# First batch's attention in four rounds of query tiles, with token chunks of 128, 128, 128 and 192 behind them

## The reference, cut to what matters

```python
# attention: batch 4, 8 heads, sequence 576, head size 64, float32
scores = q @ k.T / sqrt(64)
cum = cumsum(max(s, 0))
scores = where(causal, -1e9, scores + min(-(cum_q - cum_k), 0))
attn = softmax(scores)
x = attn @ v                                     # 2304 tokens x 512
# first dense stage, 512 -> 768 -> 512
h = max(x @ w1, x @ w2, x @ w3);  y = h @ w_out
# second dense stage, 512 -> 1536 -> 512
out = ((y @ w_a) * (y @ w_b)) @ w_out2
```

## Time and profile before

| | |
|---|---|
| median of 3 runs | 985.52 us (985.21 to 985.62) |
| the profiled execution's own time | 985.47 us |
| its span (first to last instruction) | 983.7 us |
| PE busy | 941.9 us, 96% of the span |
| DVE, ACT, POOL busy | 468.9, 406.6, 202.9 us |
| matmuls | 5776 |

### The profile page before, as it was taken

One profiled execution on the slowest core, in us unless ns is written; L12 is line 12 of the kernel. 1 busy time (PEld: TensorE's weight loads), 2 busy tenths in 40 slices (PEclk: granted clock), 3 DMA queues, 4 the chain that ended last, 5 costly groups with the idle time before them and its releaser, 6 DMA issues.

```text
span 983.7 us, 15197 instructions
## 1 busy us (share of the span) xinstructions
PE 941.9 (96%) x5776; PEld 858.7 (87%) x5776; DVE 468.9 (48%) x1054; ACT 406.6 (41%) x912; POOL 202.9 (21%) x293
## 2 busy tenths in 40 slices
PE   3688999999999999999999999999999999999998
PEld 2578899999999999999999888888888888888898
DVE  6689978877666577563323433221122112211222
ACT  4677777766655566543223333211121112111211
POOL 5556554444423324411000000000000000000000
PEclk9999999999999999999999999999999999999999
DMA  3544432222121221100032332100020001000100
GB/s 103 149 158 153 147 97 64 71 77 78 57 86 39 80 69 40 54 9 27 12 134 69 120 97 91 66 21 1 0 72 14 1 1 64 1 1 1 43 1 22
DMA packets 29240, 58.74 MB, mean 60 GB/s; under 512 B 3184, under 2 KB 15568, under 8 KB 29136
## 3 DMA queue, kind: packets, MB, share of 16 engines
q1 hardware_dynamic: 29168, 57.77, 18.6%
HBM read 47.87 MB, written 9.88 MB: 59 GB/s over the span
## 4 chain that ended last, share of the span: by engine, by line
PE 88%; DVE 5%; issue 4%; DMA 1%; POOL 1%; ACT 0%; SPq 0%; POOLq 0%; ACTq 0%; DVEq 0%
PE bank L1129 30%; PE bank L1008 21%; PE bank L1144 15%; PE bank L1027 8%; PE bank L960 5%; PE bank L990 5%; PE bank L976 4%; DVE soft L754 1%; DVE pt_lo L763 1%; DVE h_lo L794 1%; DVE qk_st L726 1%; DVE w_lo L732 1%; DMA cum_dram<-cum_row 0%; DVE qk_st L720 0%; DMA qk_raw<-in_qk 0%
## 5 line engine op out<-in xcount | busy, mean ns | idle before, releaser
L919 DVE TENSOR_TENSOR g_raw<-bank,a_sb 128x512 f32<-128x512 f32 (+1 forms) x60 | 38.3, 639 | 298.5 <-PE bank L1129 298.5
L1008 PE MATMUL bank<-xs_hi,w_hi 128*128 128x256 f32 (+1 forms) x576 | 173.9, 302 | 2.2 <-DVE xs_lo L775 1.5
L1008 PE MATMUL bank<-xs_hi,w_lo 128*128 128x256 f32 (+1 forms) x576 | 170.7, 296 | 0.0
L1008 PE MATMUL bank<-xs_lo,w_hi 128*128 128x256 f32 (+1 forms) x576 | 170.6, 296 | 0.0
L458 POOL TENSOR_SCALAR soft<-soft,rden 128x576 f32<-128x576 f32 (+4 forms) x160 | 102.7, 659 | 236.6 <-DVE rden L740 236.6
L1129 PE MATMUL bank<-y_hi,w2b_hi 128*128 128x512 f32 (+1 forms) x360 | 132.4, 368 | 0.0
L1129 PE MATMUL bank<-y_lo,w2b_hi 128*128 128x512 f32 (+1 forms) x360 | 132.4, 368 | 0.0
L1129 PE MATMUL bank<-y_hi,w2b_lo 128*128 128x512 f32 (+1 forms) x360 | 132.4, 368 | 0.0
L500 ACT ACTIVATE soft<-soft,neg_max 64x576 f32<-64x576 f32 (+4 forms) x160 | 96.1, 601 | 45.8 <-DVE neg_max L754 45.0
L1008 PEld LDWEIGHTS bank<-xs_hi,w_hi 128*128 128x128 f32 x576 | 109.3, 190 | 3.7 <-DVE xs_lo L775 1.7
L665 ACT ACTIVATE a_sb<-bank 128x512 f32<-128x512 f32 (+1 forms) x60 | 33.3, 555 | 188.5 <-PE bank L1129 188.5
(11 more groups left out here) (83 smaller groups left out, 1821.9 us busy)
## 6 DMA issues: line engine op xcount, KB each, us to landing
qk_raw<-in_qk SPq DMA_DIRECT2D x32, 576.0 KB, 3.8
w_raw<-in_w SPq DMA_DIRECT2D x40, 384.0 KB, 3.5
v_raw<-in_v SPq DMA_DIRECT2D x32, 160.0 KB, 2.2
y_raw<-y_dram SPq DMA_DIRECT2D x4, 1024.0 KB, 5.5
outT<-o_stage SPq DMA_DIRECT2D x16, 256.0 KB, 2.0
qk_raw<-in_qk SPq DMA_DIRECT2D x8, 256.0 KB, 3.1
y_dram<-m_tmp SPq DMA_DIRECT2D x8, 160.0 KB, 1.8
y_dram<-h_raw SPq DMA_DIRECT2D x8, 160.0 KB, 1.8
```

The costliest lines, as they stand in the source:

```text
L1008: ins = nc.tensor.matmul(up_ps[g][:, 0:width1(c)], up1_w(w, f, g, kc), x[:, kc, 0:width1(c)], start=(kc == 0 and at == 0), stop=(kc == KC ...
```

## The change

- The first batch's heads run in four rounds: jobs 0 to 7 take tile 0, 8 to 15 tile 1, 16 to 23 tile 2, 24 to 31 tiles 3 and 4. The full heads are jobs 32 to 55. There are 65 slots.
- The first batch's tokens become four chunks of 128, 128, 128 and 192. They start at slots 9, 17, 25 and 33, 8 slots each (`DENSE` is 4). So the fourth chunk stands beside the full heads of batch 1. The chunks of the other batches are as before, from slot 41 on, and again beside the same heads.
- q, k and v loads, copies and splits take only the keys that the round needs. A head of the first batch is loaded four times instead of twice.
- w1 has no ring: `w1_raw` has room for all pieces, in the place where `w1_lo` lies, so the low part is written over the raw one. The high copy stays on ACT; DVE subtracts 512 of 768 columns, POOL the other 256, ahead of its normalising. The pieces are spread over slots 1 to 12.
- SP loads the bias of the first 8 jobs from SBUF and no longer waits for the store of the cumulative sums at the start.
- Jobs with one tile alternate between the two score banks. In slots without dense work ACT makes the k/q copy first, and DVE splits q and k ahead of the pt subtractions.

```diff
-EARLY_TILES, LATE_TILES = (0, 1), (2, 3, 4)
+STAGES = [(0,), (1,), (2,), (3, 4)]
+PARTIAL = HEADS * len(STAGES)
+N_JOBS = PARTIAL + N_HEADS - HEADS
...
-CHUNK = [((0, SPLIT), (SPLIT, SEQ))[c % 2] for c in range(N_CH1)]
+CHUNK = [(0, P), (P, SPLIT), (SPLIT, 3 * P), (3 * P, SEQ)] + [(0, SPLIT), (SPLIT, SEQ)] * (BATCH - 1)
...
-FIRST = [9, 17, 25, 29, 33, 37, 41, 45]
+FIRST = [9, 17, 25, 33, 41, 45, 49, 53, 57, 61]
...
-DENSE = 2
+DENSE = len(STAGES)
...
-W1_PIECES = {2: [0], 4: [1], 8: [2, 3], 9: [4, 5], 10: [6, 7], 11: [8, 9], 12: [10, 11], 13: [12, 13], 14: [14, 15]}
+W1_PIECES = {n: [n - 1] for n in range(1, 8)}
+W1_PIECES.update({8: [7, 8], 9: [9, 10], 10: [11, 12], 11: [13, 14], 12: [15]})
...
+            with ExitStack() as early:
+
+                w1_raw = early.enter_context(nc.sbuf_tensor("w1_raw", [P, W1_COLS], F32))
             w1_lo = sb("w1_lo", [P, W1_COLS], F32R)
...
-            w1_raw = [sb(f"w1_raw{r}", [P, PIECE], F32) for r in range(2)]
...
-        def score_at(i):
+        def score_at(n, i):
+            if len(tiles(n)) == 1:
+                return BANK * (n % 2)
             return PARTED if i == QT - 1 else BANK * (i % 2)
...
             sp.dma_start(cum_dram, cum_row[:, :, :].bitcast(F32)).then_inc(cum_stored, 16)
-            sp.wait_ge(cum_stored, 16)
...
+            def w1_rest_sub(piece):
+                pool.wait_ge(w1_hi_done, piece + 1)
+                cols = slice(piece * PIECE + W1_SHARE, (piece + 1) * PIECE)
+                nc.gpsimd.tensor_tensor(w1_lo[:, cols], w1_raw[:, cols], w1_hi[:, cols].bitcast(F32), ALU.subtract
+                                        ).then_inc(w1_rest_done, 1)
...
                     split_v(n)
+                for piece in W1_PIECES.get(n, []):
+                    w1_rest_sub(piece)
                 if live(n):
                     for k in range(len(tiles(n))):
                         normalise(n, k)
...
             def w1_lo_sub(piece):
                 dve.wait_ge(w1_hi_done, piece + 1)
-                cols = slice(piece * PIECE, (piece + 1) * PIECE)
+                cols = slice(piece * PIECE, piece * PIECE + W1_SHARE)
...
-                if i == QT - 1 or k == 0:
+                if i == QT - 1 or k == 0 and len(tiles(n)) > 1:
                     need(pe, neg_done, TB[n] + k)
...
-                for lo, hi in ((0, SPLIT), (SPLIT, SEQ)):
-                    if lo >= last or hi <= first:
+                for lo, hi in ((first, min(last, SPLIT)), (max(first, SPLIT), last)):
+                    if lo >= hi:
                         continue
```

More of the change, by code:

```diff
@@ L62, in live, with keys @@
     return 0 <= n < N_JOBS
-N_CH1 = 2 * BATCH
-CHUNK = [((0, SPLIT), (SPLIT, SEQ))[c % 2] for c in range(N_CH1)]
+def keys(n):
+    return KEYS[tiles(n)[-1]]
+CHUNK = [(0, P), (P, SPLIT), (SPLIT, 3 * P), (3 * P, SEQ)] + [(0, SPLIT), (SPLIT, SEQ)] * (BATCH - 1)
+N_CH1 = len(CHUNK)
 WIDE = SEQ - SPLIT
@@ L73, with batch @@
 STEPS = 6
-FIRST = [9, 17, 25, 29, 33, 37, 41, 45]
+FIRST = [9, 17, 25, 33, 41, 45, 49, 53, 57, 61]
 N_SLOTS = FIRST[-1] + 4
-DENSE = 2
+DENSE = len(STAGES)
+def batch(c):
+    return max(0, (c - 2) // 2)
 def place(n):
@@ L107, in rest_of @@
     c, e = place(n)
-    return c if c is not None and e == 0 and c in (0, 1, 2, 4, 6) else None
+    return c if c is not None and e == 0 and (c < DENSE or c % 2 == 0) else None
 def ahead_of(n):
@@ L724, in split_k @@
                 dve.wait_ge(lower_done, x + 1)
-                hi = KEYS[tiles(x)[-1]]
+                hi = keys(x)
                 nc.vector.tensor_tensor(qk_st[x % 2][DH:P, 3, 0:hi], qk_raw[x % 2][DH:P, 0:hi],
@@ L1049, in ups @@
                     up_part(c, f, g)
-            scores(0, 0)
-            scores(0, 1)
+            for k in first_scores(0):
+                scores(0, k)
             def alone_slot(n):
@@ L1057, in alone_slot @@
                     transposes(m, k)
-                if tile_count(n) > 2:
-                    scores(n, 2)
                 if live(m):
                     output(m)
-                scores(n + 1, 0)
-                scores(n + 1, 1)
+                for k in first_scores(n + 1):
+                    scores(n + 1, k)
             def share(n, at):
@@ L1101, in slot @@
                     output(m)
-                if live(n + 1):
-                    scores(n + 1, 0)
-                    scores(n + 1, 1)
+                for k in first_scores(n + 1):
+                    scores(n + 1, k)
             for n in range(N_SLOTS):
```

113 lines of the change are left out of this document (58 added, 55 removed).

## The result

The changed kernel takes **1164.09 us** (median, 1163.26 to 1164.99), the kernel before 985.57 (985.21 to 985.63) on the same chip: a ratio of 1.1812 [1.1792, 1.1833], 178.5 us slower. The forecast was 1050, with a range that ended at 1068. The direction was right. The loss was 2.8 times the 64.3 us of the sum.

A forecast was written before the change was run, and what follows sets the result against it. PE was taken to bound the kernel, short of work only before 222 us. Slots 0 to 40 summed to 285.6 us against 221.3, so 985.5 + 64.3 gave 1050 us, range 1028 to 1068.

The forecast's parts named there:

- the sum: Slot lengths added up to the end of slot 40: 285.6 us against 221.3 now, +64.3, with everything behind unchanged.
- The sign: Whole kernel slower: +57 us of PE work against 63 us idle; slower by over 0.2% given 0.97.
- a matmul under some 230 columns costs 0.11 us, whatever its width: Dense matmuls of narrow chunks: the weight load's step sets 0.11 us each; up and down matmuls of batch 0 +50.4 us.
- The 0.8 for the dropped wait: Start, first slot: SP's dropped wait, less one more weight piece ahead of the loads, brings first output 0.8 earlier, at 15.6.
- the ring of 3.7: Slots 1 to 7: w1 copy, DVE and POOL subtractions in turn, normalise, transpose, copy and handovers take 3.7 us a slot.
- rival 3: Dearer handovers, and no early start from unringed w1 because POOL's share precedes normalising: about 21 us more, 1071; chance 0.17.
- the forecast's other ring: Slots 1 to 7: SP issues five loads a slot, each v load held until v is split; some 3.4 us.
- The wait behind w1: Slots 9 to 12: next transposes wait for normalising behind two w1 pieces, 2.75 us in a slot of 5.9.
- Both waits of the forecast: Slots 25 to 32: PE waits 1.1 us for DVE's mask of tile 3 and 0.8 before the output; slot 8.8.
- about 1 in eight slots: Slots with tiles 3 and 4: PE's mask waits at L960 would be about 1 us in each of eight slots.
- rival 2: Slots 17 to 40: ACT and DVE keep pace, only PE counts; 28 us less, 1022, half 1036; chance 0.16 with half.
- The clause on 81 ns: Narrow matmuls: at the skill's 81 ns, a slot's 36 would take 2.9 us, a little under a microsecond less.

The follow-up runs named there:

- wide256: Changed kernel with the dense matmuls of the first batch's four chunks run over 256 columns, the extra ones unread; 1061.45 us, ratio 1.0768.
- nowait: Kernel before, with SP's wait for the store of the cumulative sums dropped and the first 8 jobs' bias from SBUF; 985.96 us, ratio 1.0002.
- wide256_dve: wide256 with the w1 subtraction wholly on DVE and none on POOL; 1061.12 us.
- warm: Changed kernel with 24 matmuls of 512 columns, result unread, put at the start of slot 9; 1085.76 us, one run.
- wide192: Changed kernel with the dense matmuls of its 128-token chunks run over 192 columns; 1058.98 us, ratio 1.0754.
- three192: three with its middle chunk of 128 tokens run over 192 columns; 1029.16 us, ratio 1.0440.
- three: Changed kernel with three rounds (tiles 0 and 1; 2; 3 and 4) and first-batch chunks of 256, 128 and 192 tokens; 1063.76 us, ratio 1.0797.

## Why the prediction was right and wrong

**The sign** rested on one count: PE gets 57 us more work and has 63 us idle, so even without any idle time the gain is 6 us. That held in every kernel with more chunks: 1029, 1059, 1061, 1064 and 1086, all slower.

**The step that failed** is the sentence "a matmul under some 230 columns costs 0.11 us, whatever its width", and ahead of it "2.4 GHz, the granted clock of these stretches". The clock was read from stretches of 256- and 320-column matmuls and taken along to chunks of 128 columns as if it were a property of the chip. In the runs it went with the matmuls: of 864 with 128 columns nearly all took 0.213 in the changed kernel, at half the clock; padded to 256 columns, all but the first 33 ran at the high clock, save for 3.4 us. No rival had it: each varied widths, chains and handovers, at one clock. So the range had no room for it.

The table sets the forecast beside `wide256`, which has the high clock almost throughout, and the kernel after (us; outputs by time, the rest by length).

| | forecast | wide256 | after |
|---|---|---|---|
| first output | 15.6 | 16.66 | 16.47 |
| eighth output | 41.8 | 42.47 | 42.08 |
| slot 9 | 8.4 | 9.8 | 9.9 |
| slots 10 to 12, each | 5.9 | 5.7 | 9.3 |
| slots 13 to 16, each | 4.9 | 5.2 | 9.35 |
| slots 17 to 24 | 43.9 | 47.3 | 83.1 |
| slots 25 to 32 | 70.4 | 75.0 | 115.2 |
| slots 33 to 40 | 83.8 | 86.35 | 85.4 |
| end of slot 40 | 285.6 | 298.9 | 401.0 |

**Where the missing 115 us are** (401.0 less 285.6). In slots 9 to 32 there are 24 x 36 = 864 dense matmuls, at 0.213 instead of 0.11: 89 us. The rest of these slots, attention and waits, takes 89.5 us (273.5 less 864 x 0.213), where the forecast had 65.0 (160.0 less 864 x 0.11): 24.5 more. How that splits is an estimate, since busy time is modelled. The forecast's 65.0 were 43 of PE's attention work (0.9, 1.3 and 3.1 a slot) and 22 of waits. By its busy time PE was idle for 7 us of these slots. So the attention work took some 82 us, nearly twice the 43, as at half the clock, and 15 us of the waits vanished behind the slower PE. Slots 33 to 40, at the high clock, and the start add 2. That makes 115. The split between attention's own operations isn't measured.

**What the slots said point by point.**

- *First output* 16.47 for 15.6. The 0.8 for the dropped wait does not exist: `nowait` stays at 16.38. And the change's order puts the third head's load, behind the w1 piece and the store, ahead of the first output (ScalarE waits 4.28 us for it, until 14.90), which the forecast put at nothing. It read the DMA share as under 0.5 in the earlier trace rows; the row of the start has 0.52.
- *Slots alone*: 3.2 to 4.2 for the ring of 3.7, eighth output 0.3 from the forecast. So rival 3's claim that unringed w1 brings no early start is refuted. But the ring itself isn't confirmed: without POOL's share (`wide256_dve`) it should have been 3.2, and the eighth output came at 42.5 as with it. In both, ScalarE waits six times for the loads of q and k, 8.8 and 8.5 us in all. That fits the forecast's other ring, the loads' 3.4, which no run took apart, so the hit is in part luck.
- *Slot 9*: 9.9 for 8.4. The half clock explains it in the changed kernel (36 x 0.213 and 1.7 of attention, 9.4) and in `wide256` (9.8), where PE is busy for 9.0 and the clock rises only at 51.9. The wait behind w1 that the forecast had here shows as 0.8 in both.
- *Slots 13 to 24*: 4.9 and 5.3 by forecast, 4.9 to 5.0 and 5.35 in `warm`. Away from the first and last slot of a round the count of PE work was right to 0.1 us, given the clock. Slots 17 to 24 take 44.9 in all for 43.9: their first and last slot cost 2.1 on top, not 1.5.
- *Slots 25 to 32*: 8.8 by forecast, 9.1 to 9.2 at the high clock in `warm`, `wide192` and `three192`. Both waits of the forecast are there: 0.8 for the mask and 0.9 before the output, for which the profile names no releaser (`warm`, slot 26), 1.7 where the sum had 1.8. It is PE's own part that is dearer, 7.5 for 7.0. PE's waits for the mask in these slots (engine, line, waited for: us in total, times, longest), first in the kernel after, then in `wide256`:

```profile
PE bank L985 <- DVE neg_max L782: 5.5, 7, 0.8
```

```profile
PE bank L998 <- DVE neg_max L786: 5.8, 8, 0.8
```

  Seven or eight waits of up to 0.8, where I had written about 1 in eight slots. So rival 2 (only PE counts, 7.0 a slot) is refuted where the clock is high. In the changed kernel, on the other hand, PE counted alone nearly everywhere, and at twice the price.
- *Slots 33 to 40*: up 10.71 for 10.6, down 10.5 for 10.1; PE's 192-column step 0.112 for 0.11. DVE runs on without a gap but for one wait of 1.75 to 1.8 us a slot, ahead of its masks, as in the earlier trace rows.
- *Behind them*: 762.1 against 762.4 before, unchanged as said.

**What `wide256` still owes the sum** is 298.9 - 285.6 = 13.3 us. About 4.5 of it is the wider columns (above), 8 x 0.4 = 3.2 is tiles 3 and 4, 1.5 is the one drop of the clock, and the rest is the start, slot 9 and the first and last slot of tile 2. Without the wider columns that is, by estimate, a time near 1057: had the clock been as high as there, the forecast would have been some 7 us short, inside its range.

**The clause on 81 ns** that stood beside the forecast: in the Trainium skill, "TensorE: Matmul & The Clock Gate", section "Back-to-back issue gap", the sustained spacing at 128 columns is about 81 ns. This kernel's fp32r matmuls with a weight load each took 0.112 in every long stream of 128 columns here, at 2.4 GHz and unbroken for 107 us. The measurement decides: 0.11 stands. (By 81 ns a slot's 36 matmuls would have been 1.0 us cheaper, 3.96 less 2.92, not a little under one.)

**A rule that I passed over.** The same page, section "Why this matters for your kernels", advises to pad thin matmuls, since the clock otherwise falls back again and again; the section "What's actually happening" calls the low clock the default, which activity releases. The runs agree with the advice (`wide256` against the changed kernel, 103 us). The reason that the page gives for thin matmuls, waits for transfers between them, isn't what happened here: in slots 10 to 16 PE has no idle time at all and stays at 0.213. Had I worked it out from rows, it would have been a rival at the clock of the start of slot 9: 36 x 0.213 and twice the attention time in 24 slots, some 110 us on top, 1160.

**What stays open.** Why the clock rises in the last slot of tiles 3 and 4, at 314.8. Two things are new in this slot: a full head's scores, 12 matmuls of up to 512 columns instead of 6, come in beside the 128-column matmuls, and PE doesn't wait for a mask in it. No run takes them apart. Why 128 columns hold a clock that they didn't bring up. And why the same waits cost the clock in `three` after 3.7 us and in `warm` only after 30.
